# Recurrent state kept head by head on row halves, and remainder steps of two tiles issued as one pair

## The reference, cut to what matters

```
m_new = max(f + m, i);  f_stab = exp(f + m - m_new);  i_stab = exp(i - m_new)
C = f_stab * C + i_stab * outer(v, k);   n = f_stab * n + i_stab * k
y = sigmoid(o) * (C @ q) / max(|n . q|, 1)
x = y as (3072 tokens, 320)
h = x @ w_in (320 x 2048);   x = max(0.01 h, h) @ w_out (2048 x 320)
h = x @ w_in2;               out = (h * cos(h)) @ w_out2
```

## Time and profile before

| what | us |
|---|---|
| median of 3 runs (lowest, highest) | 821.76 (821.65, 822.05) |
| the profiled execution's own time | 821.87 |
| its span, first to last instruction | 820.2 |
| busy: TensorE matmul, VectorE, ScalarE, GpSimd | 809.2, 627.6, 466.7, 345.8 |
| the chain that ended last: share on TensorE | 90% |

### The profile page before, as it was taken

One profiled execution on the slowest core, in us unless ns is written; L12 is line 12 of the kernel. 1 busy time (PEld: TensorE's weight loads), 2 busy tenths in 40 slices (PEclk: granted clock), 3 DMA queues, 4 the chain that ended last, 5 costly groups with the idle time before them and its releaser, 6 DMA issues.

```text
span 820.2 us, 18114 instructions
## 1 busy us (share of the span) xinstructions
PE 809.2 (99%) x6953; PEld 785.4 (96%) x6953; DVE 627.6 (77%) x1371; ACT 466.7 (57%) x1037; POOL 345.8 (42%) x350
## 2 busy tenths in 40 slices
PE   8899999999999999999999999999999999999998
PEld 6799999999999999999999999999999999999998
DVE  7689877776777777767644588888888888888896
ACT  5365433433434334335256677777777777777776
POOL 4868445343333543433116643333333333333332
PEclk9999999999999999999999999999999999999999
DMA  9666233323223333231033501211010202020000
GB/s 290 196 203 210 81 99 120 145 83 128 80 81 128 108 127 123 89 108 66 2 116 120 170 2 49 73 38 36 3 71 1 74 1 73 1 73 1 1 25 25
DMA packets 36952, 70.10 MB, mean 85 GB/s; under 512 B 3524, under 2 KB 24068, under 8 KB 36868
## 3 DMA queue, kind: packets, MB, share of 16 engines
q1 hardware_dynamic: 36820, 68.91, 25.6%
q10 hardware_dynamic: 48, 0.05, 0.0%
HBM read 56.95 MB, written 11.99 MB: 84 GB/s over the span
## 4 chain that ended last, share of the span: by engine, by line
PE 90%; DVE 5%; POOL 2%; ACT 2%; issue 1%; DVEq 0%; POOLq 0%; ACTq 0%
PE h L698 33%; PE acc L711 13%; PE acc L713 13%; PE acc L712 12%; PE s L698 10%; PE x L674 2%; PE s L637 2%; PE s L652 2%; PE s L617 2%; DVE r_f L1299 2%; PE s L667 1%; DVE r_f L1297 1%; DVE g_f L1307 0%; POOL w_in L1525 0%; PE x L723 0%
## 5 line engine op out<-in xcount | busy, mean ns | idle before, releaser
L698 PE MATMUL h<-xT,w_in 128*128 128x384 f32 x1536 | 307.5, 342 | 1.4 <-DVE w_in L1363 0.9
L698 PEld LDWEIGHTS h<-xT,w_in 128*128 128x128 f32 x1536 | 267.8, 189 | 5.5 <-DVE w_in L1363 1.1
L871 ACT ACTIVATE t_f<-h 128x384 f32<-128x384 f32 x192 | 94.1, 490 | 279.0 <-PE h L698 278.9
L711 PE MATMUL acc<-w_out,g_hi 128*128 128x320 f32 x756 | 237.1, 314 | 0.7 <-POOL g_lo L1599 0.3
L713 PE MATMUL acc<-w_out,g_lo 128*128 128x320 f32 x756 | 233.6, 309 | 0.0
L712 PE MATMUL acc<-w_out,g_hi 128*128 128x320 f32 x756 | 232.3, 307 | 0.0
L1599 POOL TENSOR_TENSOR g_lo<-g_f,g_hi 128x384 fp32r<-128x384 f32 x123 | 126.0, 1024 | 203.9 <-ACT g_hi L871 203.9
L1287 DVE TENSOR_TENSOR g_f<-h,t_f 128x384 f32<-128x384 f32 x128 | 71.1, 556 | 112.5 <-ACT t_f L871 112.3
L711 PEld LDWEIGHTS acc<-w_out,g_hi 128*128 128x128 f32 x756 | 142.0, 188 | 2.0 <-issue 1.1
L712 PEld LDWEIGHTS acc<-w_out,g_hi 128*128 128x128 f32 x756 | 142.1, 188 | 0.0
L713 PEld LDWEIGHTS acc<-w_out,g_lo 128*128 128x128 f32 x756 | 141.8, 188 | 0.0
(11 more groups left out here) (160 smaller groups left out, 835.4 us busy)
## 6 DMA issues: line engine op xcount, KB each, us to landing
qk_s<-qk SPq DMA_DIRECT2D x24, 512.0 KB, 4.6
kvo_s<-kvo SPq DMA_DIRECT2D x24, 484.0 KB, 4.9
x_dram<-stage SPq DMA_DIRECT2D x8, 960.0 KB, 4.1
xT<-x_dram SPq DMA_DIRECT2D x8, 960.0 KB, 4.8
D<-g_dram SPq DMA_DIRECT2D x42, 128.0 KB
qe<-q SPq DMA_DIRECT2D x24, 160.0 KB, 3.0
out<-x SPq DMA_DIRECT2D x24, 160.0 KB, 1.8
eG_b<-e_dram SPq DMA_DIRECT2D x42, 80.0 KB
```

Source lines behind the costliest of these rows:

```text
L698: last = nc.tensor.matmul(bank[:, 0:BLOCK], w(a), x[:, k, :], start=(n == 0), stop=(n == 7))
L711: nc.tensor.matmul(acc[t][:, 0:DM], hi[:, r], w_out[:, 0, j, :], start=(j == 0), stop=False)
L871: copy = lambda o, i, **k: nc.scalar.activation(o, i, ACT.Copy, **k)
```

## The change

It has three parts. First, the state is kept per head on the row halves: a state matmul takes 64 rows and 64 key columns of one head (24 of them surplus) by 41 values, and writes to the row half of its own side, all into one bank; the four `scalar_tensor_tensor` of a sub-chunk take 128 rows by 41 columns; there are six state slots; the mask step, `own` and `Cm` are gone; carried matmuls take 40 rows by 41 columns, alternating row halves and banks. Second, in layer one `xT` gets a sixth part: `xT[:, 2]` holds the high parts on both row halves and `xT[:, 5]` the low parts on both, and one row half of `w_in[:, 2]` is overwritten with the low weights (`rest_lo`, on ScalarE, which half depends on the tile's parity). So `(2, 2)` gives high and low weights times the high input in one step, and what is left is high weights times low input, a step of 64 rows. Third, where a slot ends with `unit_state` (slots 4 and 9 of blocks 1 to 6), that remaining step of the next two tiles is issued as two matmuls of 64 rows, one on each row half and each into its own bank, before the two tiles begin; these tiles then have seven full steps. All other tiles of layer one have `(2, 5)` as their eighth step; layer two keeps `(5, 2)`.

The new waits: TensorE waits for `win_rest` at even slots of block 0, `unit_carried` for `F_done` in place of `C_done`, VectorE's `state` for `O_done`, the pair for `max_done` of the tile just begun.

```diff
             def load_q3(b, c):
-                sp.dma_start(qe[0:ROWS, p, :, :].rearrange("p g t -> p (g t)"),
+                sp.dma_start(qe[:, p, :, :].rearrange("p g t -> p (g t)"),
...
-                for i in range(PACK):
-                    x = e_dram[c, bass.ds(b, 1), i::PACK]
-                    n = len(range(i, HEADS, PACK))
-                    sp.dma_start(eG_b[HD * i:HD * (i + 1), p, 0:n, :], x.to_broadcast([HD, n, CHUNK])).then_inc(done, 16)
+                for e in range(2):
+                    x = e_dram[c, bass.ds(b, 1), SIDE * e:SIDE * (e + 1)].rearrange("a h t -> a (h t)")
+                    sp.dma_start(eG_b[side(e), p, :, :].rearrange("p h t -> p (h t)"),
+                                 x.to_broadcast([SUB, SIDE * CHUNK])).then_inc(done, 16)
...
             def unit_state(b, c):
+                    pe.wait_ge(pad_done, 1)
                     pe.wait_ge(kw0_done, 1)
...
                 for u in range(SUBS if c < CHUNKS - 1 else 1):
-                    for g in range(2):
+                    for h in range(SIDE):
+                        k = (SIDE * u + h) * HD
                         for e in range(2):
-                            k = (SIDE * u + PACK * g) * HD
-                            last = nc.tensor.matmul(unit_banks(b, c)[e][0:ROWS, group_cols(2 * u + g)],
-                                                    kw[side(e), c % 2, k:k + ROWS],
-                                                    v_s[side(e), c % BUFS, u, PACK * g:PACK * (g + 1), :].rearrange("p h d -> p (h d)"),
+                            last = nc.tensor.matmul(unit_banks(b, c)[0][side(e), head_cols(SIDE * u + h)],
+                                                    kw[side(e), c % 2, k:k + SUB], v_s[side(e), c % BUFS, u, h, :],
                                                     start=True, stop=True)
...
             def unit_carried(b, c):
-                pe.wait_ge(C_done, middle(b, c))
-                for g in range(GROUPS):
+                pe.wait_ge(F_done, middle(b, c))
+                for h in range(SIDE):
                     for u in range(SUBS):
...
-                        state = Cm[0:ROWS, (c - 1) % 2, 1, :] if u == 0 else Cm[0:ROWS, c % 2, 0, :]
-                        last = nc.tensor.matmul(unit_banks(b, c)[g // 2][side(u), OUT:OUT + 2 * PACK * VD][:, group_cols(g % 2)],
-                                                qe[0:ROWS, c % BUFS, g, side(u)], state[:, group_cols(g)], start=False, stop=True,
+                        state = C[:, state_slot(c, u - 1), head_cols(h)]
+                        for e in range(2):
+                            last = nc.tensor.matmul(unit_banks(b, c)[e][side(u), OUT:OUT + SIDE * VD][:, head_cols(h)],
+                                                    qe[rows_of(e), c % BUFS, h, side(u)], state[rows_of(e), :], start=False, stop=True,
...
-            def first_product(bank, x, j):
+            def first_product(bank, x, j, order):
                 w = lambda k: w_in[:, k, j * P:(j + 1) * P]
-                order = [(0, 0), (0, 3), (3, 0), (1, 1), (1, 4), (4, 1), (2, 2), (5, 2)]
...
+            FIRST_STEPS = [(0, 0), (0, 3), (3, 0), (1, 1), (1, 4), (4, 1), (2, 2)]
+
+            def begin_pair(row, i):
+
+                for t in (1, 2):
+                    pe.wait_ge(max_done, row.tile(i) + t - 1 + H_FREE)
+                    j = i % FT + t
+                    r = side(j % 2)
+                    nc.tensor.matmul(h_bank[j % 2][:, 0:BLOCK], w_in[r, 2, j * P:(j + 1) * P], xT[r, row.half(i), 5, :], start=True, stop=False)
+
+            def begins_pair(row, i):
+
+                return not row.starts(0, i) and row.unit(i, PROBS) and i % FT < FT - 2
...
                     if row.starts(0, i) and j % PT == 0:
                         pe.wait_ge(win_lo, j // PT + 1)
+                        pe.wait_ge(win_rest, j + PT)
                     pe.wait_ge(max_done, row.tile(i) - 1 + H_FREE)
-                    first_product(h_bank[i % 2], xT[:, row.half(i)], j)
+                    begun = any(j >= t and begins_pair(row, i - t) for t in (1, 2))
+                    first_product(h_bank[i % 2], xT[:, row.half(i)], j, FIRST_STEPS + ([] if begun else [(2, 5)]))
...
                 if u := row.unit(i, PROBS):
                     unit_state(*u)
+                    if begins_pair(row, i):
+                        begin_pair(row, i)
...
+            def rest_lo(k):
+
+                act.wait_ge(win_lo, k + 1)
+                for j in range(k * PT, (k + 1) * PT):
+                    copy(w_in[rest_rows(j), 2, j * P:(j + 1) * P], w_in[rest_rows(j), 5, j * P:(j + 1) * P].bitcast(F32)).then_inc(win_rest, 1)
...
+                if row.starts(0, i) and i in LATE_REST:
+                    rest_lo(LATE_REST[i])
...
             gate_weights(1)
             act.wait_ge(g_stored, 16)
             act.wait_ge(scratch, 32)
+            rest_lo(0)
+            rest_lo(1)
             over_the_row(slot)
...
             def state(b, c):
                 dve.wait_ge(U_done, unit(b, c) + 1)
+                if not first(b, c):
+                    dve.wait_ge(O_done, unit(b, c) - 1)
...
-                        for g in range(GROUPS):
-                            r = group_cols(g)
-                            last = nc.vector.scalar_tensor_tensor(C[0:ROWS, u, r], C[0:ROWS, 1 - u, r],
+                        for h in range(SIDE):
+                            last = nc.vector.scalar_tensor_tensor(now[:, head_cols(h)], C[:, state_slot(c, u - 1), head_cols(h)],
...
             def x_lo(b, c, dst):
                 dve.wait_ge(xh_done, unit(b, c) + 1)
-                split_turned(dst, turn_bank(b, c), c % TILES).then_inc(xT_done, 1)
+                r = slice(c % TILES * P, (c % TILES + 1) * P)
+                src = turn_bank(b, c)[:, 0:3 * P].rearrange("p (a t) -> p a t", a=3)
+                tt(dst[:, 3:6, r], src, dst[:, 0:3, r].bitcast(F32), ALU.subtract).then_inc(xT_done, 1)
...
-            def own_state(b, c):
...
-                own_state(*divmod(u - 1, CHUNKS))
```

More of the change, by code:

```diff
@@ L143, in build @@
         sel = x2[:, :, :].rearrange("p t d -> p (t d)")[:, 0:SIDE * CHUNK].rearrange("p (h t) -> p h t", h=SIDE)
-        pairs = x1[:, 1, 0:GROUPS * PACK * HD].rearrange("p (g n) -> p g n", g=GROUPS)
         ident_r = g_hi[:, 0, 0:P]
@@ L175, in build @@
         win_lo = sem("win_lo")
+        win_rest = sem("win_rest")
         wout_hi = sem("wout_hi")
@@ L568, in _ @@
                     wait_count(h_done, (BLOCKS + 1 + n) * FT)
-                    sp.dma_start(xT[:, half, :, :].bitcast(F32),
+                    sp.dma_start(xT[:, half, 0:5, :].bitcast(F32),
                                  x2_dram[bass.ds(n + 2, 1)].rearrange("a p c t -> (a p) c t")).then_inc(x2_in[half], 16)
@@ L692, in block_transpose @@
                 transposes(x_bank, x2[:, t, :], T2_done)
-            def first_product(bank, x, j):
+            def first_product(bank, x, j, order):
                 w = lambda k: w_in[:, k, j * P:(j + 1) * P]
-                order = [(0, 0), (0, 3), (3, 0), (1, 1), (1, 4), (4, 1), (2, 2), (5, 2)]
                 for n, (a, k) in enumerate(order):
-                    last = nc.tensor.matmul(bank[:, 0:BLOCK], w(a), x[:, k, :], start=(n == 0), stop=(n == 7))
+                    last = nc.tensor.matmul(bank[:, 0:BLOCK], w(a), x[:, k, :], start=(n == 0 and len(order) == 8), stop=(n == len(order) - 1))
                 last.then_inc(h_done, 1)
+            FIRST_STEPS = [(0, 0), (0, 3), (3, 0), (1, 1), (1, 4), (4, 1), (2, 2)]
[7 more added lines that the diff above has]
+                return not row.starts(0, i) and row.unit(i, PROBS) and i % FT < FT - 2
             def second_product(row, i):
@@ L744, in slot @@
                     pe.wait_ge(prod_done, row.tile2(i) - 3 + PROD_FREE)
-                    first_product(ring_bank[i % 4], xT[:, row.half(i)], j)
+                    first_product(ring_bank[i % 4], xT[:, row.half(i)], j, FIRST_STEPS + [(5, 2)])
                 if (u := row.unit(i, TURN)) and j < FT - 1:
@@ L816, in spread_scales @@
             def spread_scales(c):
-                for g in range(GROUPS):
-                    last = nc.tensor.matmul(scale_bank(c)[0:ROWS, g * CHUNK:(g + 1) * CHUNK], pairs[:, g, :],
+                for h in range(SIDE):
+                    last = nc.tensor.matmul(scale_bank(c)[:, h * CHUNK:(h + 1) * CHUNK], sel[:, h, :],
                                             keep_all[:, c * CHUNK:(c + 1) * CHUNK], start=True, stop=True)
@@ L889, in first_scales @@
                 act.wait_ge(eG_spread, c + 1)
-                copy(eG_b[0:ROWS, c, :, :].rearrange("p g t -> p (g t)"), scale_bank(c)[0:ROWS, :]).then_inc(eG_done, 1)
+                copy(eG_b[:, c, :, :].rearrange("p g t -> p (g t)"), scale_bank(c)[:, :]).then_inc(eG_done, 1)
             def first_state():
                 act.wait_ge(U_done, 1)
-                for e in range(2):
```

(17 more changed lines are left out.)

78 lines of the change are left out of this document (31 added, 47 removed).

## The result

The changed kernel takes **826.68 us** (median of 6 runs, 825.74 to 828.70); the kernel before, run beside it, 822.33 us (6 runs, 821.65 to 824.19). The ratio is 1.0058, with a 95% interval of 1.0041 to 1.0075: slower, by a little. The profiled run took 825.74 us over a span of 823.6, against 821.87 and 820.2, so the rows explain +3.4 us of the median's +4.35.

What follows compares the result with a forecast made beforehand. TensorE, busy 99% of the span, was taken as the bound. Start-up 2.35, block 0 1.0, blocks 1 to 6 2.0 and pairs 0.1 made +5.5 on the 820.2 us span, hence a median of 827.3; range 823.8 to 832.

Steps and rivals of the forecast that it cites:

- State: State matmuls: 32 instructions on two quarters cost 1.08 us, +0.35 a unit; +5.4 us over units 7 to 23.
- rival 2: State matmuls: the shared bank makes the row halves take turns; +0.18 a full unit, 831.5 us, up to 847; chance 0.09.
- rival 1: State matmuls: only the instruction count matters, 0.0175 us each, not the quarters; 820.4 us; chance 0.11.
- Carried: Carried matmuls: going round four quarters saves 0.19 us a unit, bounds -0.20 and -0.11; -3.4 us over units 6 to 23.
- Blocks 1 to 6: Recurrence beside the dense layer: state +5.4 and carried -3.4 give +2.0 us, with pairs +0.1 more.
- what is saved on GpSimd and VectorE is worth nothing behind 94 us, where TensorE waits for neither: From 94 us on: TensorE is busy 315.92 of 316 us, so savings on those engines count for nothing.
- Pairs: Twelve pairs, slots 4 and 9 of blocks 1 to 6: +0.01 us each, together +0.1 (-2.2 to +2.4).
- Block 0: 42 to 94 us: state +1.2, carried -0.2, VectorE's savings -0.15, ScalarE's copies +0.15; +1.0 us, bounds 0 and +1.8.
- the gain there goes into a longer wait: Block 0, carried of units 4 and 5: gain lost in the 0.7 and 0.9 us waits that VectorE's queue sets.
- Start-up: Tile 0 waits behind gate_weights(1) for two copies: +0.52 and +1.43, plus +0.4 for the chain ahead; +2.35 us.
- The costs set at nothing: Wider loads of queries and scales, new waits for O_done and F_done, everything behind 410 us: no cost.
- The rule of the Trainium skill that the prediction weighed: New state's shared bank: different row tiles can't access the same PSUM bank at the same time; the basis of rival 2.

Runs made afterwards that it cites:

- e3_four_quarters: Changed kernel with each row half's state in its own bank and odd heads on the other column half, so all four quarters are used (sums misplaced): 819.45 us.
- e4_narrow: Changed kernel with the state matmuls' weights cut from 64 to 40 key columns: 820.96 us, ratio 0.9991 to the kernel before.
- e2_own_banks: Changed kernel with row half 1's state matmuls written to bank 1 instead of bank 0 (state of heads 4 to 7 left out): 829.35 us.
- e6_no_pairs: Changed kernel without the twelve pairs, every layer-one tile with eight full steps: 823.97 us.
- e5_state_only: Changed kernel with only its new state and carried matmuls: five parts of xT, no rest_lo, no pairs: 824.90 us, ratio 1.0051 to the kernel before.
- e9_early_narrow: e1_early_rest and e4_narrow together, with weight piece 7 in slot 12 instead of 13: 815.85 us, ratio 0.9928 to the kernel before.
- e8_best: e7_early_split with 40-column state weights, weight piece 7 in slot 12, and 30 pairs instead of 12: 829.54 us, ratio 1.0093 to the kernel before.
- e10_piece4_later: e9_early_narrow with weight piece 4 rounded and subtracted in slot 5 instead of 4: 814.70 us, ratio 0.9902 to the kernel before.
- e1_early_rest: Changed kernel with rest_lo(0) and rest_lo(1) moved ahead of gate_weights(1) on ScalarE: 824.27 us, ratio 1.0031 to the kernel before.
- e11_pairs_tiny_mask: e9_early_narrow with 30 pairs and GpSimd's mask step cut to an eighth of its columns (attention weights wrong): 813.69 us.
- e7_early_split: e1_early_rest with the transfer of the scales on a semaphore of its own, waited for by its users only: 822.07 us.

## Why the prediction was right

It gave 827.3, and 826.68 was measured. The sum was +5.5 on the span, though, and the profiled runs show +3.4. By its steps:

- **State: right.** 1.08 us forecast for a unit, 1.06 measured; e3_four_quarters and e4_narrow show the reason given (each quarter has a price for new weights, whatever the others do). e2_own_banks rules out rival 2 and e3_four_quarters rival 1. The lack of any row with this pattern was made up for by L723's, which alternates between two quarters.
- **Carried: right in kind, low in size.** -0.19 forecast, with -0.20 as the bound; measured is 1.02 against 1.28, -0.26. Over 18 units this is 1.2 us more of gain.
- **Blocks 1 to 6: +2.1 forecast, -0.35 measured.** This is the largest miss. Two steps failed. The carried matmuls (above) are one. The other is "what is saved on GpSimd and VectorE is worth nothing behind 94 us, where TensorE waits for neither": e6_no_pairs against e5_state_only leaves 0.85 us, for which the merged subtraction is the likely cause. The step came from reading PE's rows alone; the waits of the weight loads in the trace of before had the 1.7 us, and the changed kernel has 0.8. These two make 2.05 of the miss of 2.45; the state's 0.32 in place of 0.35, fourteen times, is another 0.4.
- **Pairs: right.** +0.01 each forecast, +0.017 measured behind the state. A half-height step saves nothing here, because two changes of shape cost as much as the step. The gain that I expected of them later, for e6_no_pairs, wasn't there.
- **Block 0: +1.0 forecast, +1.65 measured.** The wait at tile 14 grew by 0.46 (0.92 to 1.38) where 0.45 less 0.3 was forecast: the lighter VectorE gave nothing back there. (The profile names VectorE as the one waited for; the last to end was ScalarE's pair of copies, 88.31 to 88.95 us, just ahead of tile 14 at 89.05, as forecast.) The 0.7 us at L637, whose row names no engine, are 0.38 in the changed kernel and 0.68 again in e9_early_narrow, so the 0.15 forecast there is neither borne out nor refuted. A wait that the prediction didn't have is the one of the first state matmul for `D`:

```profile
PE s L646 <- DVE D L1189: 1.4, 1, 1.4
```

  It was 0.25 us in before. The step that failed is "the gain there goes into a longer wait", which stopped at the waits that were already large. `D` stands behind a piece of `w_in` on VectorE. Before, and then the changed kernel:

```profile
50.08 1.34 DVE L1363 TENSOR_TENSOR w_in<-raw_in,w_in 128x768 fp32r<-128x768 f32 x1 [0.39 <-ACT w_in L871]
51.35 0.74 DVE L1158 TENSOR_TENSOR D<-s,D 128x256 f32<-128x256 f32 x2
```

```profile
51.88 1.05 DVE L1302 TENSOR_TENSOR g_lo<-g_f,g_hi 128x384 fp32r<-128x384 f32 x1
52.93 1.73 DVE L1393 TENSOR_TENSOR w_in<-raw_in,w_in 128x768 fp32r<-128x768 f32 x1
54.58 0.74 DVE L1189 TENSOR_TENSOR D<-s,D 128x256 f32<-128x256 f32 x2
```

  The two steps in front of `D` take 0.9 us more than in before (1.05 and 1.73 instead of 0.54 and 1.34), with steps of GpSimd beside them; that this is the collision of e8_best again is likely and not tested. With the piece a slot later, in e10_piece4_later, the wait is gone.
- **Start-up: right in the mechanism, its number partly luck.** +2.35 forecast, +2.19 measured; tile 0 starts at 37.45 (37.3 forecast), behind the copies:

```profile
37.45 2.90 PE L706 MATMUL h<-xT,w_in 128*128 128x384 f32 x8 [4.52 <-ACT w_in L896]
40.28 1.70 PE L745 MATMUL x<-ident,stage 32*64 32x16 f32 x48
```

  The turns come at 40.28, though, not 38.7: the tile's steps run at the lower clock now, 2.8 us instead of 1.43. In before the stretch lay on the steps behind the turns (38.3 to 41.7 us), so at tile 5 the sum is nearly the same. ScalarE's rows are those of the argument, the weights' step and then the copies:

```profile
36.01 0.52 ACT L937 ACTIVATE stage<-stage 32x384 f32<-32x384 f32 x1 [3.45 <-POOL stage L1524]
36.56 1.30 ACT L896 ACTIVATE w_in<-w_in 64x128 fp32r<-64x128 f32 x4
```

  e1_early_rest shows that it was the placement. Counted from ScalarE's weights step the placement cost 2.42 us, where 0.52 + 1.43 = 1.95 was forecast. The rest of the forecast, +0.4 for a longer chain ahead of it, didn't come: the weights step starts 0.24 us earlier than in before. And with the same start-up e6_no_pairs is at +0.87, 1.3 us less.
- **The costs set at nothing** were nothing: behind tile 116 the difference moves by 0.02 us.

So the total was right partly by luck. Blocks 1 to 6 were 2.45 us too dear and block 0 was 0.65 too cheap, which leaves 2 us; and the medians lie 4.35 us apart where the profiled runs lie 3.4 (span) or 3.87 (time) apart, which takes another 0.5 to 1 off the miss. A start-up that differs by 1.3 us between two profiles of the same instructions is as large as these terms.

## What to carry to other kernels

When matmuls are small, count them for each quarter of the array, by the columns of weights that the busiest quarter takes: going round all four, or leaving padding out of the weights, was worth 7 and nearly 5 us here (tile 17 to tile 116, against the changed kernel), more than the whole change costs; the 7 is from a kernel whose sums of half of the heads land where nobody reads them. When weights are split into parts on a second engine, ask of each copy what it stands behind in that engine's queue; an order of two lines was worth 2.4 us at start-up, and the slot of one subtraction another 0.9. And in a stretch where TensorE seems never to wait, look at the waits of its weight loads before a gain on another engine is set at nothing. Where one profile is compared with one other, find a stage that two profiles of the same instructions give alike, as tile 17 to tile 116 here.

## What the runs showed of the hardware

- **Quarters.** 16 rounds on two quarters cost 0.91 us above the 0.15 of entry and exit with 64 columns of weights, 0.59 with 40, and 0.45 on four quarters (8 rounds on each, 0.056 a round). The 0.15 is an estimate from the earlier trace rows; from the half units of the same traces a round is 0.058, 0.039 and 0.058 us.
- **One bank for two row halves.** The halves write different partitions of it here; with one bank or two, 1.06 us. The rule of the Trainium skill that the prediction weighed (TensorEngine Tiling (Array Packing), Restrictions and Gotchas) makes no difference between partitions; the measured time shows no turns taken. Its page PSUM — Partial Sum Buffer (PSUM bank collisions raise a hardware error) tells of an error where two row tiles write one bank and one group of 32 partitions, which isn't done here. Whether the two halves' writes ever fell in the same moment, no row shows, and at the rate of four quarters one bank wasn't tried.
- **VectorE and GpSimd.** 0.55 us became 1.65 when GpSimd's step started first, in 14 of 14 places. The Trainium skill (SBUF — State Buffer, Who interferes with whom) says that a VectorE instruction with two SBUF inputs contends with GpSimd's reads and that the first to start keeps the port; the traces agree in the order (GpSimd's mask takes 1.54 us where VectorE started first and 1.29 where it didn't), though VectorE's end at 143.37 is 0.4 us past GpSimd's at 142.96.
- **The lower clock.** Near the idle times of the start-up TensorE's granted clock was 0.50, its 1.2 GHz level, for 3.4 us in most profiles, 6.8 in three and 13.65 in e2_own_banks and e3_four_quarters; e11_pairs_tiny_mask had none, e7_early_split its only one at 84.35 us. I could not tie the length to anything in the edits. The same kernel before ranged from 819.9 to 825.1 us over 19 runs. Differences under 2 us between single runs are therefore read here from tile to tile, at full clock, and not from the totals; at tile 5 even that holds only to some 1.3 us.
- **The first matmuls.** The eight instructions at 6.8 us last 2.05 us in six of the profiles and 1.13 in the other eight, in kernels that differ little in front of them (the changed kernel and e1_early_rest not at all). The trace's first record of the granted clock (1.00) begins at 9.9 us or later in the six and at 6.3 us or earlier in the eight. Ahead of it there is none, so that they ran at the lower clock is likely and not shown.
